# One fused attention and two-layer kernel: the first two units scale their values instead of their probabilities, and the orders before the main loop change

## The chip, the cores and the metric

One core of one Trainium2 chip runs the whole kernel. The metric is the device time of one execution in microseconds (us), the median of several runs. TensorE (PE) does matmuls, VectorE (DVE) and ScalarE (ACT) read the matmul banks, GpSimd (POOL) works in on-chip memory only, SyncE (SP) issues nearly all transfers.

## The reference, cut to what matters

The reference is three stages over 2304 tokens of 512 channels. The change touches only the first.

```python
scores = scale * np.matmul(q, k.transpose(0, 1, 3, 2))      # 4 batches, 8 heads, 576 tokens, 64 wide
scores = np.where(masks, scores, -1e9)                      # heads 0-3 local (32 back), heads 4-7 strided by 32
attn = np.exp(scores - np.max(scores, axis=-1, keepdims=True))
attn = attn / (np.sum(attn, axis=-1, keepdims=True) + 1e-09)
x = np.matmul(attn, v)                                      # then 512 channels per token
h = x @ w_in                                                # 512 -> 2048, piecewise activation g(h)
y = g @ w_out                                               # 2048 -> 512
# then tokens whose skip score is positive go through one of 8 experts
```

## The kernel before, in words

The attention is cut into 32 units. A unit is one pair of heads and three or four tiles of 96 rows (local heads, 128 keys wide) or of 72 rows (strided heads, 72 keys wide). Units 0 and 1 are local, with four tiles; units 2 to 5 are strided, with four tiles. These six come before the main loop; all others are slotted into it.

The main loop has 96 steps: six chunks of 384 tokens by 16 slices of the 2048 hidden channels. Step s runs `hidden(s)` (L1010), 12 matmuls of 384 columns, and, two steps later, `output` (L1034). Each float32 product is made of three products of rounded parts: the value rounded (x_hi, win_hi) and what is left of it (x_lo, win_lo). `hidden(0)` waits for x_lo of units 0 to 3 before it starts, and for that of units 4 and 5 before its last matmuls; it also waits for the first slice of win_lo.

A unit passes through these jobs, each a letter in four lists that set the order by hand, one list for each engine:

- S, PE, `scores` (L815): q times k into two banks, one for each head. P, PE, `transpose_probs` (L838): turns the probabilities. V, PE, `values_of` (L853): probabilities times v, into one bank.
- M, DVE, `masked_scores` (L1149): scale and mask out of the banks (L1165), then the negated maximum of each row (L1169). E, DVE, `reciprocal_sums` (L1187): two row sums (L1191), one small sum (L1195) and the reciprocal (L1197). L, DVE, `rest_of_x` (L1199): x_lo (L1202).
- X, ACT, `exponentials` (L1550): for units 0 to 5 eight activations each, with the maximum as bias (L1557). C, ACT, `keep_transposed` (L1563): the turned probabilities out of their banks (L1570). H, ACT, `round_x` (L1573): x_hi (L1578). W, ACT: rounds a slice of w_in (L1617).
- G, POOL, `scale_probs` (L1718): multiplies the probabilities by the reciprocal sums (L1722). R, POOL: win_lo (L1752). `shift_scores` (L1711, L1715) subtracts the maxima; before the change it is used only for later units.

The eight banks are handed out in turn over the PE list. A job that takes a bank waits until its last user has freed it. `FILLERS` gives matmuls of a constant tile (L813) that run ahead of some PE jobs; six more run at the very start.

Of the kernel before, what the change touches and what calls it, by code (L numbers as in the profile page):

```python
# [8 lines left out]
F32 = mybir.dt.float32  # L9
# [79 lines left out]
N_PRO = 6  # L89
REST = 2  # L90
# [90 lines left out]
def bank_table():  # L181

    n_banks = {"S": 2, "P": 2, "V": 1, "Y": 1, "Z": 1, "A": 1,
# [63 lines left out]
def build(nc, qk, v, w_in, w_out, w_score_dram, w_skip, w1, w2, out):  # L247
# [4 lines left out]
    with ctx:  # L252
# [25 lines left out]
        x_hi = sb("x_hi", [P, KT, XR], F32R)  # L278
        x_lo = sb("x_lo", [P, KT, XR], F32R)

# [41 lines left out]
        warm = sb("warm", [P, 512], BF16, offset=at)  # L322
        at += 2 * 512
# [130 lines left out]
        masked_ready = sem("masked_ready")  # L454
        shift_ready = sem("shift_ready")
        exp_ready = sem("exp_ready")
        sum_steps = sem("sum_steps")
        prob_ready = sem("prob_ready")
# [115 lines left out]

        def over_tiles(u, stat):
            return stat.unsqueeze(2).to_broadcast([unit_rows(u), u.nt, unit_width(u)])

        def x_view(x, u):
# [3 lines left out]
            return row.rearrange("p (j g r) -> p g r j", g=2, r=RES_HALF)[:, u.t0 // 4]  # L582

# [225 lines left out]
        def _(pe):  # L809
            def warm_up(bank, times):  # L810

                for _ in range(times):
                    pe.matmul(bank[:, :], warm[:, 0:P], warm[:, :], start=True, stop=True)  # L813
# [24 lines left out]
            def transpose_probs(n):  # L838
# [4 lines left out]
                for hh in range(2):  # L843
# [3 lines left out]
                    pe.wait_ge(prob_ready, 2 * n + hh + 1)  # L847
# [5 lines left out]
            def values_of(n):  # L853
# [12 lines left out]
                for i in range(u.nt):  # L866
                    for hh in range(2):
# [111 lines left out]
            def do_jobs(jobs):  # L979
                for kind, n in jobs:  # L980
# [18 lines left out]
                    if kind == "P":  # L999
                        transpose_probs(n)  # L1000
                    if kind == "V":
# [64 lines left out]
            warm_up(banks[7], 6)  # L1066
# [78 lines left out]
        def _(dve):  # L1145
# [41 lines left out]
            def reciprocal_sums(n):  # L1187
                u = UNITS[n]
                for hh in range(2):
                    dve.wait_ge(exp_ready, 2 * n + hh + 1)  # L1190
                    dve.tensor_reduce(sum_terms[0:unit_rows(u), hh, 0:u.nt, 0], tiled(u, hh), AX.X, ALU.add)\  # L1191
                       .then_inc(sum_steps, 1)
                sums = row_sum[0:unit_rows(u), u.n % 8, :, 0:u.nt]
# [705 lines left out]
```

## Time and profile before

| | us |
|---|---|
| median of 3 runs (505.68 to 506.18) | 505.89 |
| the profiled execution's own time | 506.15 |
| its span in the profile | 504.3 |
| PE busy | 494.1 |
| DVE busy | 253.7 |
| POOL busy | 212.7 |
| ACT busy | 194.4 |
| first main matmul starts, from the span's start | 29.33 |

The profiled execution takes 1.85 us more than its span; that part lies outside the profile. Times below count from the start of the span. The first 29.33 us are the six first units, all the rest is the main loop and a short end.

### The profile page before, as it was taken

How to read it: one execution, taken by the hardware profiler on the slowest of the kernel's cores; microseconds unless marked ns; L12 is line 12 of the kernel's file. 1: busy time of each engine (PE TensorE's matmuls, PEld its weight loads, DVE VectorE, ACT ScalarE, POOL GpSimd, SP SyncE). 2: the span in 40 equal slices, each digit the busy share in tenths (PEclk: the TensorE clock that was granted, in tenths of full speed). 3: DMA queues.
4: the chain of work that ended last, by engine and by line, in shares of the span. 5: the costliest groups of instructions: out<-in, count | busy, mean ns of one | idle time of the engine just before them, and what ended most of it. 6: DMA issues, size and time to landing. Idle time of an engine off the chain costs nothing.

```text
span 504.3 us, 8896 instructions
## 1 busy us (share of the span) xinstructions
PE 494.1 (98%) x3427; PEld 426.6 (85%) x3427; DVE 253.7 (50%) x595; ACT 194.4 (39%) x435; POOL 212.7 (42%) x235
## 2 busy tenths in 40 slices
PE   8899999999999999999999999999999999999996
PEld 4588888889988888888888888888998898888895
DVE  5977656633335636676534666652435242332322
ACT  4974655543223324343433343433322222322222
POOL 0669877662223224465532555652222322222221
PEclk9999999999999999999999999999999999999999
DMA  8994211103001204102110421000200018840001
GB/s 270 315 388 151 73 37 45 52 2 125 1 1 48 74 23 174 51 31 60 70 48 1 173 81 34 1 2 17 106 20 1 1 22 313 292 168 1 2 1 66
DMA packets 18977, 42.15 MB, mean 84 GB/s; under 512 B 2054, under 2 KB 3920, under 8 KB 18932
## 3 DMA queue, kind: packets, MB, share of 16 engines
q1 hardware_dynamic: 18580, 41.13, 24.0%
q8 instruction: 28, 0.46, 0.4%
q10 hardware_dynamic: 256, 0.41, 0.2%
q14 instruction: 17, 0.14, 0.1%
q0 software_dynamic: 96, 0.02, 0.0%
HBM read 32.94 MB, written 8.78 MB: 83 GB/s over the span
## 4 chain that ended last, share of the span: by engine, by line
PE 89%; DVE 4%; ACT 3%; DMA 1%; issue 1%; POOL 0%; SPq 0%; DVEq 0%
PE bank L1046 39%; PE bank L1030 39%; PE bank L832 4%; PE bank L869 3%; PE bank L849 2%; ACT prob_first L1557 1%; DMA qk<-in_qk_dram 1%; PE bank L973 1%; PE bank L954 1%; DVE sum_terms L1191 1%; DVE prob_first L1165 1%; DVE prob L1181 1%; ACT g_hi L1684 0%; DVE bank L1174 0%; DVE row_max L1169 0%
## 5 line engine op out<-in xcount | busy, mean ns | idle before, releaser
L1787 POOL TENSOR_TENSOR g_lo<-act_f,g_hi 128x384 fp32r<-128x384 f32 x96 | 97.5, 1016 | 196.7 <-ACT g_hi L1684 196.2
L1675 ACT ACTIVATE act_f<-act_f,half_col 128x384 f32<-128x384 f32 x96 | 59.2, 616 | 200.7 <-DVE act_f L1414 200.7
L1414 DVE TENSOR_SCALAR act_f<-bank 128x384 f32<-128x384 f32 x96 | 53.4, 556 | 146.3 <-PE bank L1030 141.4
L1030 PE MATMUL bank<-x_hi,win_hi 128*128 128x384 f32 x384 | 87.7, 347 | 0.6 <-DVE act_f L1417 0.6
L1046 PE MATMUL bank<-wout_hi,g_hi 128*128 128x512 f32 x285 | 85.0, 406 | 0.0
L1684 ACT CAST g_hi<-act_f 128x384 fp32r<-128x384 f32 x96 | 49.2, 513 | 92.1 <-DVE act_f L1417 91.8
L1030 PE MATMUL bank<-x_hi,win_lo 128*128 128x384 f32 x384 | 83.9, 337 | 0.0
L1030 PE MATMUL bank<-x_lo,win_hi 128*128 128x384 f32 x384 | 83.1, 334 | 0.0
L1046 PE MATMUL bank<-wout_lo,g_hi 128*128 128x512 f32 x285 | 81.1, 393 | 0.0
L1046 PE MATMUL bank<-wout_hi,g_lo 128*128 128x512 f32 x285 | 81.0, 392 | 0.0
L1030 PEld LDWEIGHTS bank<-x_hi,win_hi 128*128 128x128 f32 x384 | 66.7, 188 | 8.3 <-issue 1.5
L1417 DVE TENSOR_TENSOR act_f<-act_f,bank 128x384 f32<-128x384 f32 x96 | 52.6, 547 | 36.8 <-ACT act_f L1675 33.4
L1030 PEld LDWEIGHTS bank<-x_hi,win_lo 128*128 128x128 f32 x384 | 69.6, 188 | 0.0
L1030 PEld LDWEIGHTS bank<-x_lo,win_hi 128*128 128x128 f32 x384 | 68.1, 188 | 0.1
L1046 PEld LDWEIGHTS bank<-wout_lo,g_hi 128*128 128x128 f32 x285 | 53.5, 188 | 12.6
L1046 PEld LDWEIGHTS bank<-wout_hi,g_lo 128*128 128x128 f32 x285 | 53.5, 188 | 12.3
L1046 PEld LDWEIGHTS bank<-wout_hi,g_hi 128*128 128x128 f32 x285 | 49.9, 188 | 6.9 <-issue 0.6
L1722 POOL TENSOR_TENSOR prob<-prob,row_sum 72x288 f32<-72x288 f32 (+2 forms) x52 | 37.9, 747 | 23.9 <-DVE row_sum L1197 23.9
L1715 POOL TENSOR_TENSOR prob<-prob,row_max 72x288 f32<-72x288 f32 (+1 forms) x32 | 25.7, 823 | 27.7 <-DVE row_max L1169 27.7
L1202 DVE TENSOR_TENSOR x_lo<-bank,x_hi 128x288 fp32r<-128x288 f32 (+2 forms) x32 | 18.8, 587 | 30.7 <-ACT x_hi L1578 30.5
L1191 DVE TENSOR_REDUCE sum_terms<-prob 72x4 f32<-72x288 f32 (+2 forms) x52 | 23.2, 486 | 4.9 <-ACT prob L1560 4.9
L832 PE MATMUL bank<-qk 64*96 64x128 f32 (+1 forms) x384 | 23.8, 260 | 1.6 <-DMA qk<-in_qk_dram 1.0
(130 smaller groups left out, 418.1 us busy)
## 6 DMA issues: line engine op xcount, KB each, us to landing
w_early<-in_w_dram SPq DMA_DIRECT2D x4, 2048.0 KB, 8.7
qk<-in_qk_dram SPq DMA_DIRECT2D x12, 592.0 KB, 5.0
out_dram<-y_rows SPq DMA_DIRECT2D x18, 256.0 KB, 2.6
win_raw<-in_w_in_dram SPq DMA_DIRECT2D x16, 256.0 KB, 9.7
wout_raw<-in_w_out_dram SPq DMA_DIRECT2D x16, 256.0 KB, 9.2
y_dram<-y_rows SPq DMA_DIRECT2D x15, 256.0 KB, 2.9
v<-in_v_dram SPq DMA_DIRECT2D x6, 384.0 KB
v<-in_v_dram SPq DMA_DIRECT2D x6, 288.0 KB
```

Of the source, the lines that this page charges most:

```text
L832: mm = pe.matmul(bank_of("S", n, hh)[0:rows, width * i:width * (i + 1)], buf[head, q_at:q_at + rows], buf[head, k_at:k_at + width], start= ...
L1030: mm = pe.matmul(h_ps[s % 2][:, 0:CH], w[:, f, P * k:P * (k + 1)], x[:, k, cols], start=(at == 0), stop=(at == len(order) - 1))
L1046: mm = pe.matmul(y_ps[t][:, :], g[:, s % RING, P * t:P * (t + 1)], w[:, f, :], start=(f == 0 and i == 0), stop=(f == FT - 1 and i == 2))
L1191: dve.tensor_reduce(sum_terms[0:unit_rows(u), hh, 0:u.nt, 0], tiled(u, hh), AX.X, ALU.add)\
L1202: dve.tensor_tensor(x_view(x_lo, u), values_view(bank_of("V", n), u), x_view(x_hi, u).bitcast(F32), ALU.subtract).then_inc(free_sem("V", n ...
L1414: dve.tensor_scalar(tile, h_ps[s % 2][:, 0:CH], -1.0, 1.0, ALU.max, ALU.min).then_inc(clip_ready, 1)
L1417: dve.tensor_tensor(tile, tile, h_ps[s % 2][:, 0:CH], ALU.max).then_inc(act_ready, 1)
L1675: act.activation(tile, tile, ACT.Square, bias=half_col[:, 0:1], scale=0.5).then_inc(square_ready, 1)
L1684: act.copy(g_hi[:, s % RING, :], tile).then_inc(g_hi_ready, 1)
L1715: pool.tensor_tensor(tiled(u, hh), tiled(u, hh), over_tiles(u, peak_of(u, hh)), ALU.add)\
L1722: pool.tensor_tensor(tiled(u, hh), tiled(u, hh), over_tiles(u, sums_of(u, hh)), ALU.mult)\
L1787: pool.tensor_tensor(g_lo[:, s % RING, :], act_f[:, s % 2, :], g_hi[:, s % RING, :].bitcast(F32), ALU.subtract).then_inc(g_lo_ready, 1)
```

## The change

Units 0 and 1 (`LATER = 2`) are no longer scaled on POOL. PE turns their exponentials as they are, multiplies them by v, and in the same bank also multiplies them by a column of ones, eight more matmuls a unit, which gives the row sums. DVE adds 1e-9 to these and takes the reciprocal (job E). A new PE job U (`spread_sums`) spreads the reciprocals over the 64 channels with eight matmuls; a new ACT job J copies them to x_raw, which lies where x_lo will be; a new DVE job N multiplies the values by them into x_raw; H then rounds x_raw and L subtracts x_hi from x_raw, both in on-chip memory.

For units 3, 4 and 5 (`SHIFTED = 3`) POOL subtracts the maxima (new job D), and ACT takes two whole exponentials a unit instead of eight.

The four lists are reordered, and there are fewer fillers. The constant tile is 128 wide instead of 512, read four times over, and eight instead of six matmuls of it run at the start.

```diff
-PE_BEFORE = "S0 S1 S2 S3 S4 P0 S5 P1 V0 P2 V1 P3 V2 P4 V3 P5 V4 V5"
-DVE_BEFORE = "M0 M1 E0 M2 E1 M3 M4 E2 E3 M5 E4 L0 E5 L1 L2 L3 L4 L5"
-ACT_BEFORE = "X0 X1 X2 C0 X3 C1 X4 C2 H0 X5 C3 H1 W0 H2 C4 H3 C5 H4 H5 W1 W2"
-POOL_BEFORE = "G0 G1 G2 G3 G4 G5 R0 R1 R2"
-FILLERS = {("P", 0): 4, ("S", 1): 4, ("S", 2): 9, ("P", 1): 4, ("P", 2): 5, ("P", 3): 2, ("P", 4): 2, ("P", 5): 2, ("V", 4): 2}
+SHIFTED = 3
+LATER = 2
+PE_BEFORE = "S0 S1 S2 S3 P0 S4 P1 S5 V0 V1 U0 U1 P2 P3 V2 P4 V3 P5 V4 V5"
+DVE_BEFORE = "M0 M1 M2 M3 M4 M5 E0 E1 E2 N0 E3 E4 N1 E5 L0 L1 L2 L3 L4 L5"
+ACT_BEFORE = "X0 X1 C0 C1 X2 X3 J0 X4 J1 H0 W0 X5 C2 C3 H1 H2 C4 H3 C5 H4 H5 W1 W2"
+POOL_BEFORE = "D3 D4 D5 G2 G3 G4 G5 R0 R1 R2"
+FILLERS = {("S", 1): 2, ("S", 2): 6, ("V", 0): 2, ("P", 2): 5, ("P", 3): 3, ("P", 5): 1, ("V", 4): 1}
...
-                    pe.wait_ge(prob_ready, 2 * n + hh + 1)
+                    if n < LATER:
+                        pe.wait_ge(exp_ready, 2 * n + hh + 1)
+                    else:
+                        pe.wait_ge(prob_ready, 2 * (n - LATER) + hh + 1)
...
+                if n < LATER:
+                    if n == 0:
+                        pe.wait_ge(ones_ready, 1)
+                    for hh in range(2):
+                        for i in range(u.nt):
+                            mm = pe.matmul(sums_ps(u)[:, u.nt * hh + i:u.nt * hh + i + 1],
+                                           prob_t_of(u, hh)[:, rows * i:rows * (i + 1)], ones_first[0:width, :],
+                                           start=True, stop=True)
                 mm.then_inc(full_sem("V", n), 1)
+
+            def spread_sums(n):
...
+                take_bank(pe, "U", n)
+                pe.wait_ge(sum_steps, sums_done(n))
+                for i in range(u.nt):
+                    for hh in range(2):
+                        mm = pe.matmul(bank_of("U", n)[D * hh:D * hh + D, rows * i:rows * (i + 1)],
+                                       row_sum[0:rows, u.n % 8, hh, i:i + 1].to_broadcast([rows, D]),
+                                       ident[0:rows, 0:rows], start=True, stop=True)
...
+                if n < LATER:
+                    wait_full(dve, "V", n)
+                    dve.tensor_scalar(sums, sums_ps(u).rearrange("p (h t) -> p h t", h=2), 1e-9, None, ALU.add)\
                        .then_inc(sum_steps, 1)
...
+            def scaled_values(n):
+                u = UNITS[n]
+                dve.wait_ge(factors_ready, n + 1)
+                dve.tensor_tensor(x_view(x_raw, u), values_view(bank_of("V", n), u), x_view(x_raw, u), ALU.mult)\
+                   .then_inc(free_sem("V", n), 1)
...
+                if n < LATER:
+                    dve.tensor_tensor(x_view(x_lo, u), x_view(x_raw, u), x_view(x_hi, u).bitcast(F32), ALU.subtract)\
+                       .then_inc(x_ready, 1)
+                    return
...
+                    if SHIFTED <= n < N_PRO:
+                        act.wait_ge(first_shift_ready, 2 * (n - SHIFTED) + hh + 1)
+                        a = act.activation(prob_of(u, hh), prob_of(u, hh), ACT.Exp)
...
+            def keep_factors(n):
+                u = UNITS[n]
+                wait_full(act, "U", n)
+                act.copy(x_view(x_raw, u), values_view(bank_of("U", n), u)).then_inc(free_sem("U", n), 1)
...
```

## Rows read from the trace of the kernel before

**Rows 1.** Busy time by stage: start:end, length, PE, PEld, DVE, ACT, POOL, clock, DMA.

```profile
60.00:504.00 444.00, 439.75 (x2946) 385.37 (x2944) 210.68 (x487) 155.34 (x327) 175.35 (x193) 1.00 0.18 61
```

**Rows 2.** The chain that ended last, first 32 us: start, length, what.

```profile
7.80 1.12 PE bank L832 x15
...
11.42 1.20 DVE sum_terms L1191 x2
...
17.17 2.08 ACT prob_first L1557 x8
...
25.61 0.21 DVE row_sum L1197
...
25.89 1.30 POOL prob_first L1722 x2
```

**Rows 3.** Timeline of PE: scores of units 2 to 4, values, first main matmuls.

```profile
10.90 1.78 PE L832 MATMUL bank<-qk_first 64*72 64x72 f32 x48
...
18.79 0.88 PE L869 MATMUL bank<-prob_t_first,v 128*64 128x96 f32 x16
19.61 1.25 PE L813 MATMUL bank<-warm 128*128 128x512 bf16 x5
...
28.11 1.30 PE L869 MATMUL bank<-prob_t,v_first 72*64 72x72 f32 x32
29.33 0.81 PE L1030 MATMUL bank<-x_hi,win_hi 128*128 128x384 f32 x3
```

**Rows 4.** Timeline of DVE: start, length, instruction.

```profile
16.00 0.78 DVE L1165 SCALAR_TENSOR_TENSOR prob_first<-bank,mask_s 72x288 f32<-72x288 f32 x2
...
17.42 0.81 DVE L1165 SCALAR_TENSOR_TENSOR prob_first<-bank,mask_s 72x288 f32<-72x288 f32 x2
...
20.02 0.76 DVE L1191 TENSOR_REDUCE sum_terms<-prob_first 72x4 f32<-72x288 f32 x2
...
21.13 0.78 DVE L1165 SCALAR_TENSOR_TENSOR prob_first<-bank,mask_s 72x288 f32<-72x288 f32 x2
...
23.70 0.50 DVE L1202 TENSOR_TENSOR x_lo<-bank,x_hi 128x384 fp32r<-128x384 f32 x1
```

**Rows 5.** Timeline of ACT, the exponentials of unit 1.

```profile
10.87 2.45 ACT L1557 ACTIVATE prob_first<-prob_first,row_max 96x128 f32<-96x128 f32 x8 [0.15 <-DVE row_max L1169]
```

**Rows 6.** Weight loads by form over the span: count, busy us, mean ns.

```profile
L832 PEld LDWEIGHTS bank<-qk 64*96 64x96 f32 x192 | 11.5, 166 | 5.0 <-DMA qk<-in_qk_dram 2.4 <-issue 1.5
...
L912 PEld LDWEIGHTS bank<-e_flags,e_table 128*128 128x128 f32 x4 | 0.6, 190 | 0.1
```

**Rows 7.** Timeline of weight loads near 372.6, from two narrow windows.

```profile
372.55 0.30 PEld L912 LDWEIGHTS bank<-e_flags,e_table 128*128 128x128 f32 x2
372.78 0.30 PEld L1030 LDWEIGHTS bank<-x_hi,win_hi 128*128 128x128 f32 x2
```

**Rows 8.** Timeline of DVE and POOL around 189, 214 and 377.

```profile
189.21 1.29 POOL L1715 TENSOR_TENSOR prob<-prob,row_max 72x288 f32<-72x288 f32 x2 [0.67 <-DVE row_max L1169]
...
214.47 2.03 POOL L1715 TENSOR_TENSOR prob<-prob,row_max 72x288 f32<-72x288 f32 x2 [2.79 <-DVE row_max L1169]
214.67 0.68 DVE L1319 CUSTOM_DVE_ANT_0 skip_terms<-y_rows,w_skip_sb 128x512 f32<-128x512 f32 x1
...
377.31 0.17 DVE L1234 TENSOR_TENSOR e_slot<-e_running,bank 128x12 f32<-128x12 f32 x1
377.63 1.05 POOL L1787 TENSOR_TENSOR g_lo<-act_f,g_hi 128x384 fp32r<-128x384 f32 x1 [3.57 <-ACT g_hi L1684]
377.84 0.87 DVE L1237 TENSOR_TENSOR e_slot<-e_slot,e_skipped 128x12 f32<-128x12 f32 x1
```

**Rows 9.** The slices of w_in (win_raw): issues of the first three, time to landing.

```profile
6.25 1.55 SPq L671 DMA_DIRECT2D win_raw<-in_w_in_dram  x3
...
DMA to landing us min/median/max: 7.8/9.7/11.5
```

**Rows 10.** Constant tile's matmuls (L813): durations in ns min/median/max, first and last start.

```profile
L813 PE MATMUL bank<-warm x40: 377/379/634, 1.4 to 27.8; 128*128 128x512 bf16 x40
```

More of the change, by code:

```diff
@@ L278, in build @@
         x_hi = sb("x_hi", [P, KT, XR], F32R)
+        x_lo_at = base[0]
         x_lo = sb("x_lo", [P, KT, XR], F32R)
+        x_raw = sb("x_raw", [P, KT, XR], F32, offset=x_lo_at)
         steps_at = base[0]
@@ L321, in build @@
             at += 4 * 2 * u.nt * unit_width(u)
-        warm = sb("warm", [P, 512], BF16, offset=at)
-        at += 2 * 512
+        warm = sb("warm", [P, P], BF16, offset=at)
+        at += 2 * P
+        ones_first = sb("ones_first", [P, 1], F32, offset=at)
+        at += 32
         assert at <= steps_end
@@ L457, in build @@
         sum_steps = sem("sum_steps")
+        ones_ready = sem("ones_ready")
+        factors_ready, x_raw_ready = sem("factors_ready"), sem("x_raw_ready")
         prob_ready = sem("prob_ready")
@@ L582, in x_view, with sums_ps @@
             return row.rearrange("p (j g r) -> p g r j", g=2, r=RES_HALF)[:, u.t0 // 4]
+        def sums_ps(u):
+            at = u.nt * unit_rows(u)
+            return bank_of("V", u.n)[0:unit_rows(u), at:at + 2 * u.nt]
         def values_view(ps, u):
@@ L812, in warm_up @@
                 for _ in range(times):
-                    pe.matmul(bank[:, :], warm[:, 0:P], warm[:, :], start=True, stop=True)
+                    pe.matmul(bank[:, :].rearrange("p (r n) -> p r n", n=P), warm[:, :],
+                              warm[:, :].unsqueeze(1).to_broadcast([P, 4, P]), start=True, stop=True)
             def scores(n):
@@ L1000, in do_jobs @@
                         transpose_probs(n)
+                    if kind == "U":
+                        spread_sums(n)
                     if kind == "V":
@@ L1188, in reciprocal_sums @@
                 u = UNITS[n]
-                for hh in range(2):
-                    dve.wait_ge(exp_ready, 2 * n + hh + 1)
-                    dve.tensor_reduce(sum_terms[0:unit_rows(u), hh, 0:u.nt, 0], tiled(u, hh), AX.X, ALU.add)\
+                sums = row_sum[0:unit_rows(u), u.n % 8, :, 0:u.nt]
+                if n < LATER:
+                    wait_full(dve, "V", n)
+                    dve.tensor_scalar(sums, sums_ps(u).rearrange("p (h t) -> p h t", h=2), 1e-9, None, ALU.add)\
                        .then_inc(sum_steps, 1)
-                sums = row_sum[0:unit_rows(u), u.n % 8, :, 0:u.nt]
-                dve.wait_ge(sum_steps, 4 * n + 2)
-                dve.tensor_reduce(sums, sum_terms[0:unit_rows(u), :, 0:u.nt, :], AX.X, ALU.add).then_inc(sum_steps, 1)
-                dve.wait_ge(sum_steps, 4 * n + 3)
-                dve.reciprocal(sums, sums).then_inc(sum_steps, 1)
+                else:
+                    for hh in range(2):
+                        dve.wait_ge(exp_ready, 2 * n + hh + 1)
+                        dve.tensor_reduce(sum_terms[0:unit_rows(u), hh, 0:u.nt, 0], tiled(u, hh), AX.X, ALU.add)\
+                           .then_inc(sum_steps, 1)
+                    dve.wait_ge(sum_steps, sums_done(n) - 2)
+                    dve.tensor_reduce(sums, sum_terms[0:unit_rows(u), :, 0:u.nt, :], AX.X, ALU.add)\
+                       .then_inc(sum_steps, 1)
+                dve.wait_ge(sum_steps, sums_done(n) - 1)
+                dve.reciprocal(sums, sums).then_inc(sum_steps, 1)
+            def scaled_values(n):
[3 more added lines that the diff above has]
+                   .then_inc(free_sem("V", n), 1)
+                wait_free(dve, "V", n)
+                dve.sem_inc(x_raw_ready, 1)
             def rest_of_x(n):
@@ L1406, in _ @@
                     reciprocal_sums(n)
+                if kind == "N":
+                    scaled_values(n)
                 if kind == "L":
@@ L1666, in _ @@
                     keep_transposed(n)
+                if kind == "J":
+                    keep_factors(n)
                 if kind == "H":
@@ L1774, in _ @@
             for kind, n in jobs_of(POOL_BEFORE):
+                if kind == "D":
+                    shift_scores(n)
                 if kind == "G":
```

23 lines of the change are left out of this document (18 added, 5 removed).

## The prediction

> **What bounds the kernel now.** I read the table by stage first. From 60 us on PE is busy 439.75 of 444 us [rows 1]: the main loop is PE's own work, and the change leaves it alone. So it can only move the start of the loop, 29.33 us [rows 3], and each microsecond there moves the end by as much. Second, the chain of waits up to that point [rows 2]. It starts with the scores of unit 1, which wait for their q and k and run from 7.80 to 8.92; then DVE takes over: masks and maxima of unit 1 to 11.42, then row sums (1.20 for a pair) and the masks and sums of later units. From 17.17 the chain runs through ACT's eight exponentials a unit, about 2.0 us each time, and comes back through the last sums of DVE, done at 25.82, POOL's scaling (25.89 to 27.19), the turn on PE, the values of units 4 and 5 from 28.11 [rows 3], and the first main matmul. So DVE and ACT share the bound before the loop, and PE has room there, filled in part by fillers.
>
> **The change, part by part.** I follow each engine's new list with durations of its own rows.
>
> *Up to 17 us.* The start does not move: unit 1's scores wait for the transfer. Shorter setting of the constant tile and two more of its matmuls lie ahead of the first transfer; nothing waits for them. DVE now does M2 to M5 straight after M1, from 11.42: one M of this size takes 1.42 (16.00 to 17.42) [rows 4], four make 5.7, so M5 ends at 17.1. The two local E jobs lose their sums (1.20 for one pair [rows 2], and the small sum).
>
> *PE's sums, the new long step.* The exponentials of unit 1 start at 10.87 and end at 13.32 [rows 5], so the second half of P1 runs at 13.5. S5 takes 0.6 (1.78 for three [rows 3]), two fillers 0.45 (five in 1.25), and V0 starts at about 14.85. ACT goes from these exponentials straight to the copies C0 and is done with them about a microsecond after 13.3, so it is not late. A V of this size takes 0.82 (18.79 to 19.61) [rows 3]. Behind it stand eight matmuls with 96 columns of weights and one moving column. The 16 records of L869 for eight matmuls show that a float32 product is two records [rows 3]; so these are 16 loads a unit. The price of a load with almost nothing to stream is in the flags' matmuls: starts at 372.55, 372.66 (the end of the pair, 372.85, less one load of 0.19 [rows 6, 7]) and 372.78, so 0.11 for 128 columns. The mean load grows from 166 ns at 96 columns to 190 at 128 [rows 6], 0.8 ns a column; 0.11 less 32 of these is 0.08 for 96. Sixteen make 1.3 us, V0 with its sums 2.1, V1 too. Bounds: 0.05, if such loads overlap as those of V do (0.82/16), and 0.17, if each load waits for the one before. I take 0.08, since the flags are the nearest row. V1 is then full at 14.85 + 4.2 + 0.1 = 19.15.
>
> *The stall.* DVE does E0 at once, but E1 stands in front of E2 and waits for V1 from about 17.4 to 19.15. All other M's, and X2 and X3, are done, so this is 1.75 us of idle DVE on the path. From there DVE has E1 0.3 (two small instructions), E2 to E5 four times 1.11 (20.02 to 21.13) and N0 and N1 0.50 each [rows 4]: 19.15 + 0.3 + 4.45 + 1.0 + 0.2 to the end of the last reciprocal, 25.1. Before it was 25.82. POOL and ACT keep up: D3 to D5 cost POOL 1.29 a pair [rows 8] and run from 14.0 to 18.2, before its first G; ACT loses three times 2.0 and gains three pairs of whole exponentials and two copies, eight instructions of half a microsecond or less, 4 us against 6. By its list J0 and J1 come at 20.0 and 21.1, before DVE asks for them; X5 is done at 23.2, E5 begins at 23.9. W0 moves up to 21.8 and its slice has landed by 17.8 at the latest (6.25 + 11.5) [rows 9]. No transfer is issued or moved. U0 and U1 fall into PE time that is free. A second chain (C3, H1, H2, C4, V3, P5) is only 0.05 us behind POOL's last G.
>
> *The tail.* Before, 25.82 to 29.33 are 3.51. After, one filler less (0.22) is in it: 3.3. Without more, the loop starts at 28.4, 0.9 us earlier. If PE's sums were free the start would be 26.8, for then DVE would never stand.
>
> *The port.* L0 and L1 now read two tiles of on-chip memory, where they read a bank and one tile. The trace shows what that does beside POOL. A twelve-column subtraction with one input from a bank takes 0.17; the next of its size, with both from on-chip memory, takes 0.87 and ends with POOL's instruction [rows 8]. The other way round, a pair of POOL's is 1.29 alone and 2.03 with DVE's two-tile instruction of 0.68 in it [rows 8]. So the two go one after the other. The GPSIMD Engine Reference of the Trainium skill says so in its section on specifications: POOL's memory interfaces are shared with VectorE, and instructions with two on-chip inputs contend. The trace agrees. By a rule that POOL and DVE are independent L0 and L1 would cost nothing, as cover they have 2 us. Here L0 starts at 25.0, G5 wants to start at 25.2, and P5 waits for G5 with no slack. L0 takes 0.33 of G5's time; L1 another 0.5 if it gets in between G5's halves, or it waits behind G5 and costs that nothing. So the price lies between 0 and 0.83. Where L1 waits behind all that POOL has in a row, R0 too, it ends at 28.3, L2 and L3 follow (0.6 and 0.7), and the loop starts at 29.7. I take 0.4, L0's part and a little.
>
> **Sum.** 28.4 + 0.4 = 28.8 against 29.33: the span of this execution, 504.3, becomes 503.8, its time 506.15 becomes 505.65. The median lies 0.26 below this execution; taken from it, 505.89 - 0.5 = 505.4. A measurement of this kernel tells about 0.2%, 1.0 us, from no change.
>
> **The rivals.**
>
> *The sums are cheap* (loads overlap, 0.05 or less a record). For: V's own records show such a pace [rows 3]. Against: there a record's weights are 64 columns wide (128*64), so that two can lie side by side; the sums' are 96 wide. The loop starts at 27.4 or less, and even with 0.1 for the port the time is about 504.0.
>
> *DVE's x_lo waits behind POOL.* L1 gets the port only after R0, as worked out: start 29.7, time 506.3. For it speaks the 0.87 row, against it that DVE's instruction in the 214.47 rows did not wait. This one follows the page named above, taken at its hardest for DVE.
>
> *The sums are dear*, the rival that ends slower. If a one-column product and the next load do not overlap, a record takes 0.15 to 0.17; V1 is full 2.2 to 2.9 us later than in the forecast, DVE stands as long, and the time is 507.2 to 508.2. It decides from about 0.11 a record, where the gain is gone. Against it are the flags' 0.11 at more columns.
>
> *The clock.* The constant tile's matmuls show two levels: up to 634 ns at the start, 379 at the median [rows 10], and unit 0's scores take longer than unit 1's, while the granted clock reads 1.00, the 2.4 GHz level, in every stretch I read [rows 1]. The change takes fillers away (20 for 34) and puts one-column matmuls in their place. If the engine falls to the lower level, 1.2 GHz, between 17 and 29 us, V1, P5, V4, V5 and the first main step take double: 2 to 4 us more, 508 to 509. Nothing in the rows shows a fall between 9 and 29 us, with PE idle for half a microsecond at a time.
>
> *The gain is lost later.* The first steps of the loop wait for DVE and ACT, but these follow the loop's start, and their weight slices have landed. I give it nothing of its own.
>
> **How the numbers follow.** Forecast 0.47, of it 0.05 beyond a gain of 1.0; own range 504.8 to 505.9. Cheap sums 0.27. x_lo behind POOL 0.09. Dear sums 0.10, 0.01 of it within 1.0 us. Clock 0.07. Faster by over 0.2%: 0.27 + 0.05 = 0.32. Within: 0.42 + 0.09 + 0.01 = 0.52. Slower: 0.09 + 0.07 = 0.16. The range runs from 503.7, most of the cheap case, to 507.4, the nearer end of the dear one; the clock and the tails are left out.
>
> **What would show it.** Right: V1's last record near 19.1; DVE idle some 1.7 us ahead of the second small sum; eight sum matmuls in 1.3 us; last reciprocal at 25.1; L0 or L1 longer than 0.50, or G5's pair longer than 1.3; first L1030 at 28.8. Wrong: sum records 0.05 or 0.15 apart, V matmuls of 0.88 that take more than 1.5, or a first L1030 that moves while the end does not.

## The result and the profile after

The changed kernel takes 507.57 us (506.49 to 508.10, 8 executions) where the kernel before took 505.81 (505.56 to 506.47, 8 executions): ratio 1.0030, 95% interval 1.0019 to 1.0041. It is slower by 1.8 us. The forecast was 0.5 us faster, and the range ended at 507.4. The profiled execution takes 507.42 us with a span of 505.6; before it was 506.15 and 504.3.

The table by stage comes first, as before: stage, length, busy time of PE, its loads, DVE, ACT and POOL with their counts, and then the granted clock (1.00 is the 2.4 GHz level, 0.50 the 1.2 GHz level).

```profile
16.00:18.00 2.00, 2.00 (x32) 1.99 (x32) 1.60 (x6) 1.46 (x6) 1.84 (x4) 1.00 1.01 315
18.00:20.00 2.00, 2.00 (x30) 1.87 (x28) 0.20 (x2) 0.00 (x0) 0.24 (x1) 0.96 1.09 333
20.00:22.00 2.00, 2.00 (x29) 2.00 (x26) 1.51 (x6) 0.74 (x2) 0.65 (x2) 0.50 1.02 374
22.00:24.00 2.00, 2.00 (x14) 0.89 (x11) 1.79 (x7) 1.89 (x6) 0.92 (x3) 0.69 1.03 386
24.00:28.00 4.00, 3.90 (x61) 2.91 (x58) 3.72 (x11) 3.85 (x12) 3.62 (x6) 1.00 1.05 389
...
60.00:504.00 444.00, 441.00 (x2958) 386.50 (x2956) 211.59 (x488) 156.37 (x330) 176.68 (x194) 1.00 0.17 60
```

From 60 us on PE is as busy as before (441.00 of 444 us, [rows 1] had 439.75). The difference is made ahead of the loop. There the granted clock is at the 1.2 GHz level for 3.4 us, from 19.8 to 23.2 us (worked out from the clock of the stages), and PE was busy without a break in the two microseconds ahead of that. In between 18 and 20 us DVE works 0.20 us and ACT not at all: both wait for PE.

The timeline of PE (start, length, instruction) shows what it ran:

```profile
15.14 0.88 PE L892 MATMUL bank<-prob_t_first,v 128*64 128x96 f32 x16
15.95 1.52 PE L900 MATMUL bank<-ones_first,prob_t_first 128*96 128x1 f32 x16
17.40 0.88 PE L892 MATMUL bank<-prob_t_first,v 128*64 128x96 f32 x16
18.21 1.52 PE L900 MATMUL bank<-ones_first,prob_t_first 128*96 128x1 f32 x16
19.66 2.71 PE L913 MATMUL bank<-ident,row_sum 96*64 96x96 f32 x32
22.31 1.69 PE L832 MATMUL bank<-warm 128*128 128x512 bf16 x5
...
28.75 0.42 PE L872 MATMUL bank<-ident,prob_first 72*72 72x72 f32 x4 [0.27 <-POOL prob_first L1805]
29.00 0.38 PE L832 MATMUL bank<-warm 128*128 128x512 bf16 x1
29.31 1.22 PE L892 MATMUL bank<-prob_t,v_first 72*64 72x72 f32 x32
30.46 0.79 PE L1076 MATMUL bank<-x_hi,win_hi 128*128 128x384 f32 x3
```

The sums (L900) take 1.52 us a unit, 0.095 a record; from their first start to the start of the next job it is 1.45, 0.091 a record. The spread reciprocals (L913) and the five fillers behind them run at the low clock: five fillers took 1.25 before [rows 3] and take 1.69 now. The first main matmul starts at 30.46; [rows 3] had 29.33.

DVE, with the idle time ahead in brackets:

```profile
17.51 0.16 DVE L1238 TENSOR_SCALAR row_sum<-bank 96x8 f32<-96x8 f32 x1 [0.27 <-PE bank L900]
...
19.77 0.16 DVE L1238 TENSOR_SCALAR row_sum<-bank 96x8 f32<-96x8 f32 x1 [1.87 <-PE bank L900]
...
21.69 0.56 DVE L1254 TENSOR_TENSOR x_raw<-bank,x_raw 128x384 f32<-128x384 f32 x1 [0.42 <-ACTq L1659]
...
24.67 0.50 DVE L1254 TENSOR_TENSOR x_raw<-bank,x_raw 128x384 f32<-128x384 f32 x1
25.31 0.81 DVE L1243 TENSOR_REDUCE sum_terms<-prob_first 72x4 f32<-72x288 f32 x2
...
26.36 0.20 DVE L1249 RECIPROCAL row_sum<-row_sum 72x8 f32<-72x8 f32 x1
26.48 0.97 DVE L1263 TENSOR_TENSOR x_lo<-x_raw,x_hi 128x384 fp32r<-128x384 f32 x2
```

DVE stands 1.87 us ahead of the second unit's sums (forecast 1.75), then 0.42 ahead of N0, and ends its last reciprocal at 26.56 (25.1). N1 (24.67) is a row of 0.50, but the next instruction starts 0.64 us after it. POOL's last scaling lies beside L0 and L1:

```profile
26.64 1.96 POOL L1805 TENSOR_TENSOR prob_first<-prob_first,row_sum 72x288 f32<-72x288 f32 x2 [0.38 <-DVE row_sum L1249]
28.56 1.27 POOL L1835 TENSOR_TENSOR win_lo<-win_raw,win_hi 128x512 fp32r<-128x512 f32 x1
```

It takes 1.96 where a pair takes 1.29 alone [rows 8].

### The profile page after: what moved, and what is told of

Read it like the earlier page. It is cut to its first block, busy times and chain, and to the rows that moved or that the text cites. A ratio compares the mean times of both kernels' runs of the same rounds, so it can differ in the third digit from the quotient of the medians.

```text
span 505.6 us, 8991 instructions
## 1 busy us (share of the span) xinstructions
PE 497.6 (98%) x3479; PEld 431.2 (85%) x3479; DVE 251.9 (50%) x594; ACT 191.7 (38%) x419; POOL 213.2 (42%) x237
## 4 chain that ended last, share of the span: by engine, by line
PE 92%; DVE 4%; ACT 3%; issue 1%; POOL 0%; DVEq 0%; ACTq 0%
PE bank L1092 39%; PE bank L1076 39%; PE bank L852 4%; PE bank L892 4%; PE bank L872 3%; ACT prob_first L1627 1%; PE bank L832 1%; PE bank L1017 1%; PE bank L998 1%; DVE sum_terms L1243 1%; PE bank L900 1%; DVE prob L1227 1%; ACT g_hi L1767 0%; DVE bank L1220 0%; DVE row_max L1225 0%
## 5 line engine op out<-in xcount | busy, mean ns | idle before, releaser
L1805 POOL TENSOR_TENSOR prob<-prob,row_sum 72x288 f32<-72x288 f32 (+2 forms) x52 | 37.9, 748 | 23.2 <-DVE row_sum L1249 23.1
L1266 DVE TENSOR_TENSOR x_lo<-bank,x_hi 128x288 fp32r<-128x288 f32 (+1 forms) x30 | 17.6, 587 | 30.9 <-ACT x_hi L1652 30.8
L1243 DVE TENSOR_REDUCE sum_terms<-prob 72x4 f32<-72x288 f32 (+2 forms) x52 | 23.2, 487 | 4.9 <-ACT prob L1630 4.9
L1840 POOL TENSOR_TENSOR wout_lo<-wout_raw,wout_hi 128x512 fp32r<-128x512 f32 x16 | 20.6, 1287 | 11.2 <-ACT wout_hi L1702 11.2
```

The source lines that it names most:

```text
L1805: pool.tensor_tensor(tiled(u, hh), tiled(u, hh), over_tiles(u, sums_of(u, hh)), ALU.mult)\
L1840: pool.tensor_tensor(wout_lo[:, f, :], wout_raw[:, f, :], wout_hi[:, f, :].bitcast(F32), ALU.subtract)\
```

## The experiments

Two theories at first. **Clock:** with fewer fillers, or with one-column products in their place, TensorE falls to its lower level in some stretch, in a part of the executions. **Waits:** the time is DVE's stall for PE's sums, their price, and the port. All fourteen runs in one table. The fourth column counts executions whose mean granted clock over the whole span is 0.995 or less, of how many, and then the lowest and highest; 0.001 is half a microsecond of clock, or one microsecond spent at the low level. The mean also counts the idle end of the span, where most of the traces show the low level again (2.1 us of it in e10_after_wide, 2.9 in e12_before_wide); there it costs nothing and takes up to 0.003 off the mean. The last is the start of the first main matmul in the profiled execution.

| run | median us | ratio to before [95%] | at 0.995 or less; clock | first main matmul |
|---|---|---|---|---|
| the changed kernel | 507.57 | 1.0030 [1.0019, 1.0041] | 5 of 8; 0.993 to 0.998 | 30.46 |
| e1_keep_awake | 508.97 | 1.0040 [1.0024, 1.0057] | 5 of 9; 0.991 to 1.000 | 32.53 |
| e2_before_few_fillers | 508.63 | 1.0039 [1.0023, 1.0054] | 12 of 12; 0.985 to 0.993 | 32.33 |
| e3_scale_only | 511.99 | 1.0111 [1.0091, 1.0130] | 4 of 4; 0.982 to 0.990 | 34.48 |
| e4_l2_first | 507.59 | 1.0022 [1.0013, 1.0031] | 6 of 12; 0.993 to 1.000 | 29.21 |
| e5_in_bank | 506.86 | 1.0014 [1.0004, 1.0024] | 2 of 12; 0.993 to 1.000 | 29.17 |
| e6_e2_ahead | 507.43 | 1.0028 [1.0017, 1.0038] | 5 of 12; 0.992 to 0.997 | 31.05 |
| e7_all_three | 508.51 | 1.0044 [1.0029, 1.0059] | 6 of 12; 0.992 to 1.000 | 33.37 |
| w1_wide_sums | 510.64 | 1.0089 [1.0073, 1.0105] | 6 of 6; 0.988 to 0.993 | 32.35 |
| v2_act_sums | 504.05 | 0.9954 [0.9941, 0.9968] | 0 of 6; 0.998 to 1.000 | 27.64 |
| e8_wide_ones | 506.82 | 1.0006 [0.9996, 1.0016] | 0 of 12; 0.998 to 1.000 | 29.29 |
| e9_shift_only | 505.75 | 0.9989 [0.9978, 1.0000] | 0 of 12; 0.996 to 1.000 | 29.20 |
| e10_after_wide | 506.96 | 1.0014 [1.0002, 1.0026] | 1 of 12; 0.992 to 1.000 | 29.83 |
| e11_before_columns | 510.00 | 1.0068 [1.0049, 1.0088] | 2 of 6; 0.995 to 0.998 | 32.43 |
| e12_before_wide | 511.14 | 1.0097 [1.0082, 1.0111] | 2 of 4; 0.995 to 0.998 | 30.71 |

The kernel before, beside these on four occasions, had medians of 506.21 to 506.46 and never a clock under 0.996 in 95 executions. The limit of 0.995 misses most of the shorter falls: the changed kernel's profiled execution, with its fall of 3.4 us, reads 0.996 and is not among the 5. At 0.997 or less are 7 of 8 executions of the changed kernel, 10 of 12 of e4_l2_first, 10 of 12 of e5_in_bank and all of e6_e2_ahead, but 1 of 24 of e8_wide_ones and e10_after_wide together. Of the kernel before it is 33 of 95; none of these was profiled, and they are no slower than its others (505.65 to 506.59 us), so where they lost clock is not known. The ratios are what to compare, and a first main matmul of one profiled execution stands for that execution only.

**The fillers alone.** The kernel before with the changed kernel's fillers:

```diff
-FILLERS = {("P", 0): 4, ("S", 1): 4, ("S", 2): 9, ("P", 1): 4, ("P", 2): 5, ("P", 3): 2, ("P", 4): 2, ("P", 5): 2, ("V", 4): 2}
+FILLERS = {("S", 1): 2, ("S", 2): 6, ("V", 0): 2, ("P", 2): 5, ("P", 3): 3, ("P", 5): 1, ("V", 4): 1}
```

> The kernel before, with the changed kernel's fillers (20 instead of 34) and nothing else. If the missing fillers let the clock fall: a granted clock below 1.00 somewhere between 12 and 29 us and a median 0.5 to 2 us above the 505.8 of before. If the one-column sums do it: clock 1.00, median 505.5 to 505.9, since the fillers of before stand partly in PE's idle time.

Measured: 2.3 us slower in the median (1.0039, which is 2.0 us), and low in every execution. The table by stage, PE alone (stage, length, busy, clock):

```profile
14.00:16.00 2.00, 0.68 (x6) 0.97 1.04 291
16.00:18.00 2.00, 1.97 (x21) 0.50 1.08 358
18.00:20.00 2.00, 1.88 (x10) 0.50 1.10 340
28.00:30.00 2.00, 1.73 (x22) 0.89 1.05 386
30.00:32.00 2.00, 2.00 (x31) 0.50 1.06 388
```

After a stretch with PE busy 0.68 of 2 us the clock falls. Fillers cost PE time and do no work, but the old order can't do with the 20 of the new one. This is the clock theory's, in the old order.

**More fillers in the new order.** Two ahead of V1 and two ahead of U0:

```diff
+FILLERS = {("S", 1): 2, ("S", 2): 6, ("V", 0): 2, ("V", 1): 2, ("U", 0): 2, ("P", 2): 5, ("P", 3): 3, ("P", 5): 1, ("V", 4): 1}
```

> The changed kernel with two fillers more ahead of V1 and two ahead of U0, inside the stretch in which PE has only one-column products. Theory A (the granted clock falls at about 19.9 us because PE streams almost nothing in the sums, and that costs 1.2 us in the median): the clock reads 1.00 from 16 to 30 us, U0 and U1 take 1.6 us together instead of 2.7, the runs lie within 0.5 us of one another, median 506.0 to 506.8. Theory B (the sums' own time and the wait of E1 behind them are the cost, the clock is a side effect): the four fillers only add 0.4 to 0.9 us, median 508.0 to 508.5.

Measured: no gain, and a median of 508.97 that neither theory gave. In the profiled execution the clock is full to 28 us (U0 and U1 take 1.54 us together, not 2.71) and falls later:

```profile
26.00:28.00 2.00, 2.00 (x44) 1.00 1.06 392
28.00:30.00 2.00, 1.57 (x16) 0.73 1.05 387
30.00:32.00 2.00, 2.00 (x28) 0.50 1.05 385
```

The executions lie apart: 505.2 to 506.2 at 0.999 and 1.000, 507.1 to 509.0 at 0.991 and 0.993 (the numbers are spans). So where the clock holds, this kernel is no faster than before (507.07 to 508.01 us, beside a median of 506.32), and it does not hold reliably. Fillers in these places are no cure.

**One part alone: the scaling without POOL's subtractions.**

```diff
-SHIFTED = 3
-POOL_BEFORE = "D3 D4 D5 G2 G3 G4 G5 R0 R1 R2"
+SHIFTED = 6
+POOL_BEFORE = "G2 G3 G4 G5 R0 R1 R2"
```

> The changed kernel without the subtraction on POOL: ACT does eight exponentials a unit for units 3 to 5 again. If POOL's subtraction is worth what it takes from ACT, E4 and E5 wait for X4 and X5, each some 1.3 us later, and the median is 509 to 510. If DVE's wait for V1 hides it, the first main matmul moves by under 0.5 us and the median stays at 507.4 to 508.

Measured: 5.6 us slower than before, more than either expectation, with the clock low from 19 to 26 us and again from 29 us. ACT is late too: DVE waits 1.18 and 0.53 us for its exponentials at 26.36 and 27.34. So the subtractions on POOL are worth those waits in the new order; how much of the rest is the clock's is not separated.

**The port.** First by order, one L from a bank ahead of L0 and L1:

```diff
-DVE_BEFORE = "... E3 E4 N1 E5 L0 L1 L2 L3 L4 L5"
+DVE_BEFORE = "... E3 E4 N1 E5 L2 L0 L1 L3 L4 L5"
```

> The changed kernel with L2 ahead of L0 and L1 on DVE, so that the two subtractions with both inputs in on-chip memory no longer stand beside G5. If they hold up POOL: G5's pair takes 1.3 to 1.5 us instead of 1.96, the last values and the first main matmul come 0.3 to 0.6 us earlier, median 507.0 to 507.3. Rival (the cost only moves into POOL's next piece, R0, for which the main loop waits too): no change, 507.4 to 507.8.

Measured: the same median as the changed kernel's, a ratio of 1.0022 beside 1.0030, with intervals that overlap. The pair of G5 is back at 1.29, but the contention moves on to R0:

```profile
26.23 2.13 DVE L1263 TENSOR_TENSOR x_lo<-x_raw,x_hi 128x384 fp32r<-128x384 f32 x2
...
26.28 1.67 POOL L1835 TENSOR_TENSOR win_lo<-win_raw,win_hi 128x512 fp32r<-128x512 f32 x1
```

The two subtractions take 2.13 instead of 0.97, and the first main matmul waits 0.95 us for x_lo. The executions of this run also bear on what the clock is worth: the two at 0.998 or more took 506.01 and 506.46 us, the ten below 507.26 to 508.01. The 506.01 is the profiled one, and its first transfers are also the earliest of all profiles. Then by data: N writes its product back into V's bank, so that H and L read a bank, as they did before, and the banks are handed out so that this bank stays free of others.

```diff
-                dve.tensor_tensor(x_view(x_raw, u), values_view(bank_of("V", n), u), x_view(x_raw, u), ALU.mult)\
+                dve.tensor_tensor(values_view(bank_of("V", n), u), values_view(bank_of("V", n), u), x_view(x_raw, u),
+                                  ALU.mult).then_inc(x_raw_ready, 1)
```

> The changed kernel with N's product written back into V's bank; H reads it there, and L0 and L1 have one input in a bank again. The banks after P3 are handed out so that nobody waits for the two that are held longer. If L0 and L1 with both inputs in on-chip memory cost time by holding up POOL or waiting for it: L0 and L1 take 0.50 us each, G5's pair 1.29 instead of 1.96, and from the start of V0 to the first main matmul there are 14.2 to 14.7 us where the changed kernel has 15.3 (at the same clock); median 506.7 to 507.2. Rival (POOL's loss is hidden by the wait for the values): no difference, 507.4 to 507.8.

Measured: 1.0014, as if half of the loss were gone, but the intervals overlap and fewer executions show a long fall of the clock (2 of 12). G5 takes 1.29 again and three L's take no more than three alone:

```profile
25.64 2.05 DVE L1260 TENSOR_TENSOR x_lo<-bank,x_hi 128x384 fp32r<-128x384 f32 x3
...
25.80 1.29 POOL L1799 TENSOR_TENSOR prob_first<-prob_first,row_sum 72x288 f32<-72x288 f32 x2 [0.18 <-DVE row_sum L1249]
```

From the last reciprocal to the first main matmul there are 3.45 us, and 3.90 in the changed kernel: the port costs 0.45. The edit does more than that: with the product in the bank, N0 and N1 take 0.45 us each up to the next start, where they take 0.64 to 0.70 in the changed kernel, and from V0 to the first main matmul there are 13.89 us, fewer than the 14.2 to 14.7 expected. Not all of it arrives at the end. In step 0 PE stands 0.57 us, up to 31.04, put down to issue, so the profile names no cause; e8_wide_ones, with the same edit in it, stands 0.76 us in the same step, up to 31.15. That stays open.

**The stall.** E2 ahead of E1, so that DVE has work while PE makes the second unit's sums:

```diff
-DVE_BEFORE = "M0 M1 M2 M3 M4 M5 E0 E1 E2 N0 E3 E4 N1 E5 L0 L1 L2 L3 L4 L5"
+DVE_BEFORE = "M0 M1 M2 M3 M4 M5 E0 E2 E1 N0 E3 E4 N1 E5 L0 L1 L2 L3 L4 L5"
```

> The changed kernel with E2 ahead of E1 on DVE. If DVE's wait of 1.87 us for the sums of unit 1 is on the path: the last reciprocal before the main loop comes 1.0 to 1.1 us earlier, median 506.4 to 506.9. If PE's own chain (sums, U0, U1, fillers, P2) or the clock sets the pace: under 0.3 us, 507.3 to 507.8.

Measured: nothing gained. The wait is cut and comes back in front of N0, since the spread reciprocals need the same sums (and here ran at the low clock, 2.83 us):

```profile
19.85 0.16 DVE L1241 TENSOR_SCALAR row_sum<-bank 96x8 f32<-96x8 f32 x1 [1.12 <-PE bank L903]
...
21.89 0.56 DVE L1257 TENSOR_TENSOR x_raw<-bank,x_raw 128x384 f32<-128x384 f32 x1 [1.65 <-ACTq L1662]
...
26.56 0.20 DVE L1252 RECIPROCAL row_sum<-row_sum 72x8 f32<-72x8 f32 x1
```

The clock was low for 6.8 us in this execution, twice as long as in the changed kernel's, and a part of the wait for U0 is its doing; but the seven executions at 0.996 or 0.997 took 507.01 to 507.44 us, no less than the changed kernel's at such a clock. The bound is a loop through three engines (V1, its sums, E1, U, J, N), not DVE's list. Next, this order, the product in the bank and more fillers together:

```diff
-FILLERS = {("S", 1): 2, ("S", 2): 6, ("V", 0): 2, ("P", 2): 5, ("P", 3): 3, ("P", 5): 1, ("V", 4): 1}
+FILLERS = {("S", 1): 4, ("S", 2): 6, ("P", 1): 2, ("V", 0): 2, ("V", 1): 2, ("U", 0): 2, ("P", 2): 5, ("P", 3): 3, ("P", 4): 2, ("P", 5): 2, ("V", 4): 2}
```

> Both edits (product in the bank, E2 ahead of E1) with 32 instead of 20 fillers. If the granted clock costs what the other two do not: clock 0.998 to 1.000 in most runs, and a median of 505.5 to 506.3, level with the kernel before. If the fillers cost as much as the clock: 507 or more.

Measured: 1.0044, and half of the executions still at a low clock. In the profiled one the fall starts at about 19.6, inside the sums of V1, and lasts 6.8 us:

```profile
18.99 2.24 PE L903 MATMUL bank<-ones_first,prob_t_first 128*96 128x1 f32 x16
```

The first main matmul moves to 33.37, by this fall and by fillers that stand in PE's queue ahead of work that others wait for. And another way to get sums already spread, a matmul with 64 columns of ones as weights and the probabilities streaming, DVE taking the reciprocal of the whole 128x384 block (lists and fillers are changed to suit):

```diff
+                    mm = pe.matmul(bank_of("U", n)[D * hh:D * hh + D, 0:cols], ones_first[0:unit_width(u), :],
+                                   prob_t_of(u, hh), start=True, stop=True)
...
+                dve.reciprocal(x_view(x_raw, u), values_view(bank_of("U", n), u)).then_inc(factors_ready, 1)
```

> Another way to the same values: the ones are the weights (64 columns), the turned exponentials stream over them 384 columns wide, so that the sums come out spread over the 64 channels in two matmuls a unit; DVE takes the reciprocal of the spread sums (0.5 us) and multiplies in the bank. No one-column products, no U matmuls by the identity, no copy J, no wait of E behind V. The 1e-9 is not added (the sum is at least 1). PE streams in the place where it only loaded weights. If the sums' form and the wait behind them were the fault: first main matmul at 26.5 to 27.5 us, median 503.5 to 504.5. If the clock falls all the same: 0.99 or less, median 505 to 507.

Measured: 1.0089, slower than either expectation. The reciprocal, expected at 0.5 us, is what fails:

```profile
19.58 2.50 DVE L1243 RECIPROCAL x_raw<-bank 128x384 f32<-128x384 f32 x1
```

The subtraction of the same shape takes 0.50 [rows 4]. PE then waits 3.37 us for DVE ahead of P4, and the clock falls.

**The one-column products.** They stream one column for each load. Here they stream 64 columns of ones into U's bank, with the same loads. First on top of e5_in_bank:

```diff
-                            mm = pe.matmul(sums_ps(u)[:, u.nt * hh + i:u.nt * hh + i + 1],
+                            mm = pe.matmul(sums_ps(u)[:, D * (u.nt * hh + i):D * (u.nt * hh + i + 1)],
```

> The changed kernel with N's product written back into the bank (as in the run e5_in_bank), and the sum matmuls stream 64 columns of ones into U's bank instead of one column into V's. The loads are the same, so a pair costs PE little more (64 columns are about as long as a load). If the one-column products are what lets the granted clock fall: clock 1.00 in every stretch to 30 us in most executions and a median of 506.0 or less against e5_in_bank's 506.86. If the removed fillers and the other gaps decide: executions still lie between 0.993 and 1.0 of granted clock, median 506.7 to 507.3.

Measured: 0.998 to 1.000 in all twelve executions, where e5_in_bank had 0.993 to 1.000, and 1.0006, no different from before. But the median, 506.82, is not the 506.0 expected and no better than e5_in_bank's 506.86; a gain in time is not shown by this pair. Then the same single edit in the changed kernel itself:

> The changed kernel with one thing altered: the sixteen sum products stream 64 columns of ones, not one, into U's bank. Weight loads, counts, lists and fillers are the changed kernel's. If the one-column products let the granted clock fall: 0.998 to 1.000 in nearly all executions, first main matmul at 29.8 to 30.2 (0.96 us earlier than 30.46 from U0 and U1 at full clock, less the start of the transfer) and median 506.7 to 507.0 beside a before of 505.8 to 506.4. If the fewer fillers do it: 0.993 to 0.998 as in the changed kernel, median 507.4 to 507.8.

Measured: eleven of twelve at 0.998 or above, where the changed kernel has one of eight, and 1.0014 where it has 1.0030; these two intervals overlap. The timeline of PE against the changed kernel's, then the start of E1 and the last reciprocal on DVE:

```profile
18.08 1.57 PE L900 MATMUL bank<-ones_first,prob_t_first 128*96 128x64 f32 x16
19.58 1.54 PE L913 MATMUL bank<-ident,row_sum 96*64 96x96 f32 x32
21.05 1.25 PE L831 MATMUL bank<-warm 128*128 128x512 bf16 x5
...
29.83 0.79 PE L1076 MATMUL bank<-x_hi,win_hi 128*128 128x384 f32 x3
...
19.69 0.16 DVE L1238 TENSOR_SCALAR row_sum<-bank 96x8 f32<-96x8 f32 x1 [1.92 <-PE bank L900]
...
25.73 0.20 DVE L1250 RECIPROCAL row_sum<-row_sum 72x8 f32<-72x8 f32 x1
```

Streaming 64 columns costs 0.05 us a unit (1.57 for 1.52), and U0 and U1 come out 1.17 us shorter. The count of fillers is still 20, so in the new order the fall hangs on the one-column products, at that count. One thing goes with them: the wide products are written into U's bank, the narrow ones into V's, and no run separates the two. Last, the products added to the kernel before, with all its 34 fillers, read by nobody: with one column,

```diff
+                if n < 2:
+                    for hh in range(2):
+                        for i in range(u.nt):
+                            at = u.nt * rows + u.nt * hh + i
+                            mm = pe.matmul(bank_of("V", n)[0:rows, at:at + 1],
+                                           prob_t_of(u, hh)[:, rows * i:rows * (i + 1)], ones_first[0:width, :],
+                                           start=True, stop=True)
```

> The kernel before with all its 34 fillers; PE makes the eight one-column sum products behind V0 and V1 and nobody reads them (1.5 us of PE each, in time that PE has free up to the 1.2 us fillers ahead of P2). If one-column products let the clock fall by themselves: granted clock 0.993 to 0.997 in half of the executions or more, median 1 us or more above the next kernel's. If a fall needs the missing fillers as well: 0.997 to 1.000 as before, median within 0.4 us of the next kernel's, both at 0 to 1.5 us over before.

and the same with 64 (`at:at + D` for `at:at + 1`, `ones_first` as wide):

> As the kernel ahead of it, but the products nobody reads stream 64 columns of ones: the control, with as many loads and as long a stretch of PE. Either way the clock stays at 0.997 to 1.000 and the time is that of before plus what the longer V0 and V1 push back, 0 to 1.5 us.

The table by stage of the first, and then of the second:

```profile
18.00:20.00 2.00, 1.67 (x25) 1.00 1.10 343
20.00:22.00 2.00, 1.76 (x16) 0.75 1.05 384
22.00:24.00 2.00, 2.00 (x11) 0.50 1.05 386
24.00:26.00 2.00, 2.00 (x29) 0.90 1.05 386
```

```profile
18.00:20.00 2.00, 1.85 (x27) 1.00 1.07 322
20.00:22.00 2.00, 1.95 (x18) 1.00 1.04 375
22.00:24.00 2.00, 2.00 (x33) 1.00 1.03 368
24.00:26.00 2.00, 2.00 (x29) 1.00 1.05 386
```

In these two profiles the clock falls behind V0's products with one column, even with all fillers, and does not with 64 columns, and the loop starts at 32.43 and 30.71. That is one execution of each. Over the executions the two are not told apart (0.995 to 0.998 each; the second's longer idle end alone brings it to 0.997), and the expectations on the medians failed. The control is 1.4 us later than before, as allowed, but another 3 us come behind its work: its last DVE instruction starts at 503.13 and its span ends at 508.8, where it is 501.69 and 504.3 before. Why is open, so neither median is used. That one-column products lower the clock rests on the 24 executions of e8 and e10 beside the 20 of e5_in_bank and the changed kernel, and on where the falls start: in the changed kernel, e3, e6 and e7 at 18.9 to 19.8 us, inside V1's one-column products or 0.1 us behind them.

**The other part alone, and a version without the sums on PE.** The kernel before with the maxima of units 4 and 5 subtracted by POOL, nothing else moved:

```diff
+SHIFTED = 4
-POOL_BEFORE = "G0 G1 G2 G3 G4 G5 R0 R1 R2"
+POOL_BEFORE = "G0 G1 D4 G2 G3 D5 G4 G5 R0 R1 R2"
```

> The kernel before with one part of the change alone, for units 4 and 5: POOL subtracts the maxima (two pairs of 1.29 us, placed after G1 and after G3), ACT takes two whole exponentials for each instead of eight. All other orders and all 34 fillers as before. DVE keeps its work (it ends its last reciprocal at 25.8), so if DVE bounds the stretch the first main matmul stays within 0.4 us of 29.3 and the median at 505.6 to 506.2; if ACT's exponentials bound it, 28.0 to 28.6 and a median of 504.8 to 505.3; if POOL's new pairs push G4 and G5 back, 30 or later and 506.6.

Measured: 0.9989, with an interval that ends at 1.0000: about half a microsecond gained and just not clear of noise, with the first main matmul at 29.20 in place of 29.33. DVE keeps its list, and with it the bound. On top of that ACT makes the row sums of units 0 and 1 as it makes their exponentials, so DVE loses two sums for each unit, and the lists follow:

```diff
+SUMMED = 2
+DVE_BEFORE = "M0 M1 E0 M2 M3 E1 M4 E2 M5 E3 E4 L0 E5 L1 L2 L3 L4 L5"
+ACT_BEFORE = "X0 X1 X2 C0 X3 C1 X4 H0 X5 C2 H1 C3 W0 H2 C4 H3 C5 H4 H5 W1 W2"
+POOL_BEFORE = "G0 G1 D4 G2 D5 G3 G4 G5 R0 R1 R2"
+FILLERS = {("S", 1): 4, ("S", 2): 9, ("P", 0): 4, ("P", 1): 6, ("V", 0): 6, ("P", 2): 3, ("P", 3): 2, ("P", 4): 1, ("P", 5): 1}
+                                a = act.activation(tile, tile, ACT.Exp, bias=peak_of(u, hh)[:, i:i + 1],
+                                                   accum_out=sums_of(u, hh)[:, i:i + 1])
```

> The kernel before, with the row sums of units 0 and 1 taken by ACT as a by-product of their exponentials (two DVE sums of 0.6 us and the small sum fall away for each of these units), the maxima of units 4 and 5 subtracted by POOL (ACT then takes two whole exponentials for each instead of eight), orders to suit, 36 fillers. No one-column products, no spread reciprocals, no second unit waiting behind PE. Theory A (what counts is DVE's and ACT's work ahead of the loop, with the fillers kept so that the clock stays at the 2.4 GHz level): first main matmul at 27.1 to 27.6 against 29.33, median 503.5 to 504.5. Theory B (the accumulation makes each exponential longer, by 0.25 us or more): first main matmul at 29.3, median 505.8 to 506.2. Theory C (the clock falls whatever is done when this stretch is reordered): clock under 0.9 in some stretch between 16 and 36 us, median over 506.5.

Measured: 504.05 us, ratio 0.9954 [0.9941, 0.9968]. It beats both kernels. Each sum is a record of 0.19 us on ACT that overlaps the exponentials: sixteen of these take 6.18 us with their sums (8.56 to 14.74) and 4.83 without (in the changed kernel), 0.08 us a sum. DVE ends its last reciprocal at 23.67 (25.82 before), and the clock holds (0.998 to 1.000) with 36 fillers. How the gain is shared between the sums, the subtractions and the order is not separated; the subtractions alone gave about 0.5 of the 2.3 us. Its timeline, ACT first and then PE:

```profile
8.56 0.40 ACT L1573 ACTIVATE prob_first<-prob_first,row_max 96x128 f32<-96x128 f32 x1 [5.64 <-DVE row_max L1176]
8.87 0.19 ACT L1573 ACTIVATION_READ_ACCUMULATOR prob_first<-prob_first,row_max 96x1 f32 x1
...
27.64 0.80 PE L1037 MATMUL bank<-x_hi,win_hi 128*128 128x384 f32 x3
```

## Why the prediction was wrong

Two steps failed. The clock was put at nothing in the sum, and it cost 0.55 us at the start of the loop. The terms of the path up to the loop (V0's start, the sums, N0 and N1, the tail) were too small by 1.11 us together. Either is enough to use up the forecast gain of 0.53.

Its steps, with the changed kernel and the same kernel at full clock (e10_after_wide) beside them, one execution each. Ends are starts plus lengths of the rows.

| step, us | forecast | changed kernel | at full clock |
|---|---|---|---|
| V0 starts | 14.85 | 15.14 | 14.96 |
| V1 and its sums are full | 19.15 | 19.73 | 19.65 |
| DVE idle ahead of E1 | 1.75 | 1.87 | 1.92 |
| DVE idle ahead of N0 | 0 | 0.42 | 0 |
| from V1 full to the last reciprocal's end | 5.95 | 6.83 | 6.28 |
| last reciprocal ends | 25.1 | 26.56 | 25.93 |
| pair of G5 | over 1.29 | 1.96 | 1.97 |
| from there to the first main matmul | 3.7 | 3.90 | 3.90 |
| first main matmul | 28.8 | 30.46 | 29.83 |

- **The bound.** Right: only the start of the loop moves. The start is 1.66 us later than forecast, and this execution's time 1.77.
- **The clock: the first step that failed.** It was a rival with a chance of 0.07, with its place between 17 and 29 us. The profiled execution shows it there, and five others read a lower mean clock still: at least 6 of 8. "Nothing in the rows shows a fall between 9 and 29 us" was true, but those were rows of a kernel with fillers in its gaps, and they could not show what happens without them. The products with one column were counted as time on PE and not as work of another kind. The rival's own size was too large: what ran at the low level was U0, U1 and a part of the five fillers, not V1, P5, V4 and V5, and DVE hid a part. From V1 full to the last reciprocal it costs 0.55 us (6.83 less 6.28); the other 0.08 between 30.46 and 29.83 was there before the fall. Between the ratios of e10_after_wide and the changed kernel it is 0.0016, 0.8 us, not clear of noise by itself; in e4_l2_first the two executions at a full clock and the ten others lie 0.8 us or more apart.
- **The path: the second step that failed.** V0's start is 0.29 late: by the starts of the rows the second half of P1 takes 0.45, S5 0.68 and two fillers 0.53, where 0.3, 0.6 and 0.45 were taken. V0, V1 and their sums take 4.59, not 4.3, another 0.29. The sums are 0.091 a record from start to start, not 0.08 (the row alone is 0.095, and 0.098 with 64 columns): the row of the flags was the nearest one, but subtracting 0.8 ns a column from it went too far. Cheap and dear sums were both wrong in size. But the 0.11 from which "the gain is gone" leaves out the port: with the forecast gain of 0.53 over 32 records it is gone from 0.097. By the same numbers the dear rival's time starts at 507.6 and not at 507.2.
- **DVE's list.** The stall was as forecast. At full clock the jobs behind it take 6.28 for 5.95. It is N0 and N1: rows of 0.50, but 0.65 each up to the next start in e10_after_wide, where 0.50 was taken. All of it is on the path, because there is no slack behind the last reciprocal.
- **The port.** Right in kind and size: 0.4 taken, 0.45 measured by e5_in_bank, G5's pair stretched from 1.29 to 1.96. By the Trainium skill, GPSIMD Engine Reference, section "1. Specifications", VectorE's instructions with two on-chip inputs contend with POOL; the trace agrees, and e4_l2_first shows the other half, DVE stretched to 2.13 by POOL's R0. x_lo did not wait behind all of POOL's work, so that rival fell.
- **The sum.** 1.66 is 0.55 of clock, 0.58 to V1 full, 0.33 of DVE's jobs and 0.20 of tail. With the clock held the kernel would still be 0.7 us slower than before (1.0014 [1.0002, 1.0026]), and not 0.5 faster; that is inside the range and on the side given 0.52 for no change. With the fall the median, 507.57, lies 0.17 beyond the range.

What stays open: why e1_keep_awake and e7_all_three fall in half of their executions with more fillers (at 28.9 and at 19.6 us in the profiled ones), while e8 and e10 with 20 hardly do; where the kernel before loses clock in a third of its executions; the 0.57 and 0.76 us in step 0 of e5_in_bank and e8_wide_ones; and the 3 us at the end of e12_before_wide.

## What to carry to other kernels

A kernel that holds its clock with filler matmuls has no rows that show what the clock does without them: when an edit removes or replaces some, give the fall a real chance and a price in the sum, not a remote one, and read the mean clock of every execution, for one profile can show any of them. Here a busy PE was not enough, so count what it streams; a product with one column is a load with almost nothing behind it. Take prices from start to start, not from the length of a row: 0.65 for 0.50, twice, was 0.3 of the 1.11 us that the path was short of. And before a sum goes to another engine over a loop of three hand-offs, see whether an engine that already reads the data can give it as a by-product: here ACT did for 0.08 us a sum what cost PE 0.18 us a sum (eight in 1.45), DVE a stall of 1.87 and the clock.

## What the runs showed that was not expected

- The granted clock fell with PE busy 2.00 of 2.00 us ahead of it, loads and one-column products. It read 0.997 or less in 7 of 8 executions of the changed kernel and in 1 of 12 when its products had 64 columns, in 10 of 12 of e5_in_bank and in none of 12 with 64 columns there. One kernel's executions differ: 0.991 to 1.000 in e1_keep_awake. The Trainium skill, TensorE: Matmul & The Clock Gate, Part 1, says that the same kernel shows a different number of slow matmuls from run to run, depending on where the clock gate stands when the kernel starts. It says so of a kernel's first matmuls; in the profiles here the falls start at 15.9 us or later, so no run here shows just that.
- A reciprocal costs 0.20 us for 72x8 and 2.50 us for 128x384, 6.5 ns an element, five times the subtraction of that shape. The Trainium skill, VectorE: DVE Perf Modes, says in "First, the fixed hardware budget" that a reciprocal repeats a divide step eight times; it gives no time, and a price well above the subtraction's fits that.
- The time of the first transfers moves from execution to execution: unit 1's scores start at 6.38 us in e4_l2_first's profile and at 8.11 in e1_keep_awake's, with the same code ahead of them. Spans of the kernel before lie between 503.1 and 505.9 at a mean clock of 0.999 or 1.000, and a start that moves by 1.73 us could be a part of that, but not all. It is as much as the loss measured here, so a single profile of each kernel decides nothing at this size.
